# Seven instead of twelve attention steps ahead of the first matmul layer, and keys times values in four array quarters

## The reference, cut to what matters

```python
# q, k, v: 4 batches, 8 heads, 576 positions, 64 features; g_norm: 64
kv  = einsum('bhsd,bhse->bhde', k, v)            # 64 x 64 per head
out = einsum('bhsd,bhde->bhse', q, kv)
x   = out / sqrt(mean(out * out, -1) + 1e-6) * g_norm     # -> 2304 tokens x 512
x   = ((x @ w_a) * (x @ w_b)) @ w_out                      # layer 1, d_ff 1536
y   = (sigmoid(x @ w_gate) * (x @ w_val)) @ w_out2         # layer 2
```

## Time and profile before

| what | value |
|---|---|
| median of three runs | 886.71 us |
| profiled execution | 886.38 us, span of the trace 884.6 us |
| TensorE busy in the span | 870.4 us, 98% |
| VectorE busy | 646.0 us, 73% |
| ScalarE busy | 511.2 us, 58% |
| granted TensorE clock | full in all 40 slices |
| data moved | 189.81 MB, mean 215 GB/s |

### The profile page before, as it was taken

The page is one execution under the profiler, slowest core; times in us unless marked ns, Lnnn a source line. Parts: engine busy times, 40 slices in busy tenths (PEclk is TensorE's granted clock), DMA queues, the critical chain, the costliest instruction groups (busy, mean ns, idle before and its releaser), DMA issues.

```text
span 884.6 us, 16335 instructions
## 1 busy us (share of the span) xinstructions
PE 870.4 (98%) x5843; PEld 844.2 (95%) x5843; DVE 646.0 (73%) x1260; ACT 511.2 (58%) x1031; POOL 18.9 (2%) x69
## 2 busy tenths in 40 slices
PE   7999999999999999999999999999999999999998
PEld 5878999999999999999999999988999999999998
DVE  2688889872877893768994888982787894676773
ACT  3776655553565574555575556563666574656453
POOL 1122000000000000000000000000000000000000
PEclk9999999999999999999999999999999999999999
DMA  9843588886565682345583578788457486435276
GB/s 331 286 161 108 181 307 266 272 292 203 195 204 204 216 304 87 128 155 212 182 276 120 201 265 291 283 289 300 150 202 265 173 288 176 154 131 208 92 239 190
DMA packets 99344, 189.81 MB, mean 215 GB/s; under 512 B 6976, under 2 KB 48704, under 8 KB 99264
## 3 DMA queue, kind: packets, MB, share of 16 engines
q1 hardware_dynamic: 99184, 188.71, 63.4%
q10 hardware_dynamic: 80, 0.07, 0.0%
HBM read 146.28 MB, written 42.47 MB: 213 GB/s over the span
## 4 chain that ended last, share of the span: by engine, by line
PE 92%; DVE 3%; ACT 2%; DMA 1%; issue 1%; SPq 1%; POOL 0%; DVEq 0%; ACTq 0%; POOLq 0%
PE bank L893 58%; PE bank L979 10%; PE bank L977 10%; PE bank L929 6%; PE bank L932 4%; PE bank L828 1%; PE bank L805 1%; PE bank L791 1%; DMA q_in<-in_q_dram 1%; DMA wo<-wo_dram 1%; PE bank L841 1%; DVE x_lo L1429 1%; SPq L552 1%; ACT x_hi L1113 0%; DVE sum_sq L1325 0%
## 5 line engine op out<-in xcount | busy, mean ns | idle before, releaser
L893 PE MATMUL bank<-x_hi,w_hi 128*128 128x384 f32 x1008 | 340.1, 337 | 1.8 <-DVE c_a L1579 0.8
L893 PE MATMUL bank<-x_hi,w_lo 128*128 128x384 f32 x1008 | 337.9, 335 | 0.0
L893 PE MATMUL bank<-x_lo,w_hi 128*128 128x384 f32 x1008 | 337.4, 335 | 0.0
L893 PEld LDWEIGHTS bank<-x_hi,w_hi 128*128 128x128 f32 x1008 | 189.2, 188 | 7.3 <-issue 2.3
L893 PEld LDWEIGHTS bank<-x_lo,w_hi 128*128 128x128 f32 x1008 | 189.3, 188 | 2.3
L893 PEld LDWEIGHTS bank<-x_hi,w_lo 128*128 128x128 f32 x1008 | 189.2, 188 | 0.0
L1145 ACT ACTIVATE h_parts<-h 128x384 fp32r<-128x384 f32 x184 | 95.7, 523 | 81.3 <-PE bank L979 25.0
L1424 DVE TENSOR_TENSOR w_lo<-s_raw,w_hi 128x512 fp32r<-128x512 f32 x144 | 98.9, 687 | 50.2 <-ACT w_hi L1099 49.9
L1424 DVE TENSOR_TENSOR w_lo<-w_raw,w_hi 128x512 fp32r<-128x512 f32 (+1 forms) x144 | 79.5, 552 | 73.0 <-ACT w_hi L1099 73.0
L1465 DVE TENSOR_TENSOR h_parts<-h,h_parts 128x384 fp32r<-128x384 f32 x184 | 100.0, 552 | 22.3 <-ACT h_parts L1145 22.0
L1226 ACT ACTIVATE bank<-bank 128x384 f32<-128x384 f32 x72 | 34.2, 476 | 103.9 <-PE bank L893 103.9
(11 more groups left out here) (94 smaller groups left out, 822.6 us busy)
## 6 DMA issues: line engine op xcount, KB each, us to landing
wo<-wo_dram SPq DMA_DIRECT2D x60, 512.0 KB, 4.8
s_raw<-s_dram SPq DMA_DIRECT2D x48, 512.0 KB, 4.5
wo<-wo_sums_dram SPq DMA_DIRECT2D x48, 512.0 KB, 4.4
s_dram<-s_raw SPq DMA_DIRECT2D x24, 512.0 KB, 4.7
wo_dram<-wo SPq DMA_DIRECT2D x24, 512.0 KB, 5.3
wo_sums_dram<-h_parts SPq DMA_DIRECT2D x12, 1024.0 KB, 7.5
w_raw<-in_moe_w_a_dram SPq DMA_DIRECT2D x18, 512.0 KB, 3.6
w_raw<-in_moe_w_b_dram SPq DMA_DIRECT2D x18, 512.0 KB, 3.5
```

Source lines behind the costliest of these rows:

```text
L893: last = pe.matmul(to[:, 0:HT], w[:, u % 2, at, c, :], xx[:, i, c, :], start=(OPENS[i] and c == 0 and n_pass == 0), stop=(c == 1 and n_pas ...
```

## The change: what it does

1. Seven steps run in front instead of twelve. The thirteen others stand between the products of units 0 to 7, one every 15/4 slots. Keys times values of batches 2 and 3 move into slots 10 and 18 (`KV_LATE_AT`); their copies stand one slot later.
2. Keys times values takes two head pairs at a time and writes all four 64x64 quarters of the array: `tile_position=(i * DH, c * DH)` instead of `(i * DH, i * DH)`. There are as many matmuls as before. The copies are 64 wide in partition halves, four instructions per engine instead of two.
3. Loads: the weights of unit 0 come first of all, and are split first of all; batch 1's queries come in two parts; batch 3's keys and queries come in unit 0.
4. Unit 0 takes its products in the order 0, 3, 1, 2, 4, 5, 6; products 0 and 3 stand among the last back transposes of the seven steps. The operands are made in the same order.
5. The output steps of tile 0 start at unit 8 with two per unit, so ten first results are kept instead of four, the later ones in `t_raw`. The weight sums of tile 0 are three jobs instead of four, those of tile 1 three instead of two.

```diff
-    LATE = 12
-    KV_PIECE_AT = {0: ((0, 2),), 1: ((0, 3),), 2: ((1, 0),), 3: ((1, 1), (1, 2)), 4: ((1, 3),),
...
+    LATE = 7
+    KV_PIECE_AT = {1: ((0, 1),), 4: ((1, 0), (1, 1))}
...
+    QUERY_BEHIND = {1: (2, 3), 2: (4,), 4: (5, 6)}
+    X_BEHIND = {3: (0,), 4: (1,), 6: (2, 3)}
...
-    X_FIRST = (0, 3, 5, 1, 2, 4, 6)
-    T_SUMS_AT = {10: (0,), 11: (1,), LATE: (2,), LATE + 1: (3,)}
-    X_LO_AT = {8: (0,), 9: (3,), 10: (5,), 11: (1,), LATE: (2,), LATE + 1: (4,), LATE + 3: (6,)}
+    X_FIRST = (0, 3, 1, 2, 5, 4, 6)
+    T_SUMS_AT = {LATE + 1: (0,), LATE + 3: (1,), LATE + 4: (2,), LATE + 5: (3,)}
+    X_LO_AT = {5: (0,), LATE: (3,), LATE + 2: (1,), LATE + 3: (2,), LATE + 4: (4, 5), LATE + 5: (6,)}
...
-    QUERY_AT = {0: 12, 2: 13, 4: 14, 6: 15, 8: 16, 10: 17, 12: 18, 14: 19}
+    KV_LATE_AT = {10: 2, 18: 3}
+    QUERY_AT = {4 + 15 * n // 4: LATE + n for n in range(ALL_STEPS - LATE)}
+    ATTEND_AT = {k + 1: s for k, s in QUERY_AT.items()}
+    X_AT = {k + 5: s for k, s in QUERY_AT.items()}
+    OUT_FROM = 8
...
                 for r in range(R):
-                    for i in range(2):
-                        half = slice(i * DH, (i + 1) * DH)
-                        keys, values = [kv_in[half, pair_, which, r * DH:(r + 1) * DH] for which in range(2)]
-                        last = pe.matmul(kv_bank(b, i, pair_)[half, pair_ * DH:(pair_ + 1) * DH], keys, values,
-                                         start=(r == 0), stop=(r == R - 1), tile_position=(i * DH, i * DH))
+                    for c in range(2):
+                        for i in range(2):
+                            half = slice(i * DH, (i + 1) * DH)
+                            keys, values = [kv_in[half, 2 * group + c, which, r * DH:(r + 1) * DH] for which in range(2)]
+                            last = pe.matmul(kv_bank(b, i)[c * DH:(c + 1) * DH, group * DH:(group + 1) * DH], keys, values,
+                                             start=(r == 0), stop=(r == R - 1), tile_position=(i * DH, c * DH))
...
+            product(0, 0, 0)
+            transpose_x(LATE - 3)
+            transpose_x(LATE - 2)
+            product(0, 0, 3)
+            transpose_x(LATE - 1)
...
-        SUMS_AT = ({3: 0, 5: 1, 7: 2, 9: 3}, {1: 4, 4: 5}, {})
+        SUMS_AT = ({6: 0, 8: 1, 10: 2}, {1: 3, 3: 4, 5: 5}, {}, {3: 0, 5: 1, 7: 2, 9: 3}, {1: 4, 4: 5}, {})
```

More of the change, by code:

```diff
@@ L779, in transpose_q @@
                 b, group, quarter = place_of(s)
-                if not rest(s):
-                    pe.wait_ge(q_loaded[b % 2][group], 32 * (b // 2 + 1))
+                if b == 1:
+                    pe.wait_ge(q_loaded[1][0 if quarter == 0 and not rest(s) else 1], 16 * HEAD_PAIRS)
+                elif not rest(s):
+                    pe.wait_ge(q_loaded[b % 2][group], q_loads(b))
                 before = before_in_bank(qT_place, s)
@@ L1019, in _ @@
                         if i:
-                            for _ in range(2):
-                                next(behind, None)
-                    for _ in behind:
-                        pass
+                            for _ in range(2 * len(behind)):
+                                next(behind[(i - 1) // 3 * (len(behind) - 1)], None)
                 if fast(tau):
@@ L1070, in prepare @@
             def prepare(at):
-                for g in W_HI_AT.get(at, ()):
-                    split_w(0, g)
+                for u, g in W_HI_AT.get(at, ()):
+                    split_w(u, g)
                 for n in X_HI_AT.get(at, ()):
@@ L1193, in _ @@
             for s in range(LATE):
-                i = s % STEPS
+                if s:
+                    root(s - 1)
                 square(s)
-                if i + 2 < STEPS and s + 2 < LATE:
-                    copy_q(s + 2)
-                if i == STEPS - 1 and s + 1 < LATE:
-                    copy_q(s + 1)
-                root(s)
-                for b, pairs in KV_COPY_AT.get(s, ()):
-                    copy_kv(b, pairs)
-                if s >= LAG:
-                    write_x(s - LAG)
-                if i == STEPS - 1 and s + 2 < LATE:
-                    copy_q(s + 2)
-                prepare(s)
+                for ahead in X_BEHIND.get(s, ()):
+                    write_x(ahead)
+                prepare(s)
+                for b, groups in KV_COPY_AT.get(s, ()):
+                    copy_kv(b, groups)
+                for ahead in QUERY_BEHIND.get(s, ()):
+                    copy_q(ahead)
+            root(LATE - 1)
+            write_x(LATE - 3)
+            prepare(LATE)
+            seed(0, 0)
+            write_x(LATE - 2)
+            prepare(LATE + 1)
+            write_x(LATE - 1)
+            for i in range(2, FIRST):
+                prepare(LATE + i)
             for tau in range(ALL_TILES):
@@ L1528, in _ @@
                     invert(s - 1)
+                sum_squares(s)
                 prepare(s)
-                sum_squares(s)
-                for b, pairs in KV_COPY_AT.get(s, ()):
-                    copy_kv(b, pairs)
+                for b, groups in KV_COPY_AT.get(s, ()):
+                    copy_kv(b, groups)
                 if s:
                     normalise(s - 1)
+            invert(LATE - 1)
+            prepare(LATE)
+            prepare(LATE + 1)
+            normalise(LATE - 1)
+            for i in range(2, FIRST):
+                prepare(LATE + i)
             for tau in range(ALL_TILES):
```

395 lines of the change are left out of this document (239 added, 156 removed).

## The result

The changed kernel took 894.88 us (median of 4 runs, 893.7 to 898.77), the kernel before 886.56 us on the same chip (885.08 to 886.91): a ratio of 1.0105 (95% interval 1.0071 to 1.0138). The forecast was 887.0 us with a range of 882.5 to 892.5; the time is outside, on the slow side.

A forecast was written before the change was run, and what follows sets the result against it. TensorE was taken as bound, nearly without gaps, at full clock; some 10 of 886 us in play. 886.38 + 1.5 + 5.0 - 1.2 + 0.8 - 5.8 = 886.7 us, plus 0.33 for the median: 887.0 us, range 882.5 to 892.5.

The forecast's parts named there:

- four quarters, -5.8 us: Keys times values: four array quarters take 19 ns per record instead of 29.2, over eight 72-record pieces; between 0 and -8.4.
- the page cited in the prediction: Trainium skill page: some 60 cycles overhead per matmul, 25 ns, which would make the keys times values term -2.4 us.
- The relay: Unit 0's first products wait for operands handed on by VectorE and ScalarE, cover moved away; stage's gaps cost +5.0 us.
- Gaps 10.3 us: TensorE's summed waits from the first attend to product 6 of unit 0, against 5.3 us before.
- The prediction's second mechanism: VectorE and ScalarE set the pace of unit 0's first products once the steps covering them move; stage costs +5.0 us.
- The start, +1.5 us: Up to the first attend: unit 0's weights load ahead, so it starts at 12.8 us, before at 11.32.
- Units 8 on, at nothing: Later output steps in tile 0 were taken as hidden by units running from loaded weights, at no cost.
- +0.8 us between the products: Moved steps between products: slower matmuls behind transposes and waits for kv copies, less 0.5 us idle; +0.8 us.
- four quarters at full rate: Faster rival for keys times values: 14.6 ns per record, 884.4 us; chance 0.26.
- rate kept: Slower rival for keys times values: four quarters run no faster than two, 29.2 ns per record, 892.8 us; chance 0.15.

The follow-up runs named there:

- column halves apart: Changed kernel with keys times values run through its nine blocks for one pair, then the other, so never two column halves at work: 898.55 us, ratio 1.0123.
- third warm-up: Changed kernel with three wide warm-up matmuls in place of two ahead of the first piece of keys times values: 893.04 us, ratio 1.0073.
- changed again: The changed kernel run once more, unaltered: 896.35 us, ratio 1.0107; its profiled execution took 896.50 us.
- all three repairs: Changed kernel with third warm-up, 28 throw-away matmuls in the first products' gaps, and first two output steps split ahead of weight sums in unit 7: 892.71 us, ratio 1.0065.
- The filler: Changed kernel with 28 throw-away matmuls of 384 columns issued in the gaps of unit 0's first products: 894.54 us, ratio 1.0091.
- the run with a step inside the relay: Changed kernel with attention step 7 pulled into the gaps of unit 0's first products, later steps each one place earlier: 898.12 us, ratio 1.0128.

## Why the prediction was wrong

**The supply of instructions.** The step that failed most is "four quarters, -5.8 us". The rate was better than taken: 16.8 ns a record where 19 was chosen, which would have been (29.2 - 16.8) x 576 records = 7.1 us. What reaches the end is some 2 us in the changed kernel, by a difference that is not clear of noise (the run with column halves apart), and in the kernel before 1.6 us in the profiled execution and nothing in the median (888.23 against 886.64). Stops take back much of the rest, and they come from TensorE's own stream of instructions.

*Their place is a record number.* 2 records more moved them by 2, 28 by 28, 16 by 16. TensorE's records from its first one up to the stop, in the changed kernel, with the third warm-up and in the kernel before with four quarters (columns: busy us of TensorE, clock, DMA share, GB/s):

```profile
0.00:25.00 25.00, 17.20 (x343) 1.00 0.91 325
0.00:24.50 24.50, 18.45 (x343) 1.00 0.92 331
0.00:24.50 24.50, 18.42 (x343) 1.00 0.93 333
```

In eight of the profiles a stop stands behind exactly 343 records, in two different orders of the work, and the one in batch 2's piece behind 712, in all six profiles that have it. An instruction queue (q8) is in the trace, one packet of 16 KB at a time, and such a packet lies inside the long stop of the changed kernel's second profile (24.16 to 27.29 us; the window is 24.5 to 25.0 us):

```profile
q8 instruction: 1, 0.02, 12.0%
```

*Their end is the packet's.* Read from the traces, in us:

| kernel, stop behind | TensorE has run out | the packet starts | TensorE goes on | behind the packet's start |
|---|---|---|---|---|
| changed, 343 | 26.41 | 26.86 | 29.18 | 2.32 |
| changed again, 343 | 24.16 | 24.89 | 27.29 | 2.40 |
| third warm-up, 343 | 23.77 | 22.43 | 24.74 | 2.31 |
| all three repairs, 343 | 23.70 | 21.98 | 24.40 | 2.42 |
| all three repairs, 960 | 73.56 | 74.34 | 76.67 | 2.33 |
| kernel before, 843 | 51.58 | 50.19 | 52.48 | 2.29 |

The packets and the places come in step, one for one. Over the fourteen profiles the first eight packets belong to 27 stops called "issue", and each of these ends 2.1 to 2.8 us behind the start of its packet; where no stop stands, TensorE gets to the place 2.1 us or more behind it (the places of single records are good to a few). So the length of a stop is what is left of these 2.3 us or so when TensorE has run out. It is short where the packet started early (0.70 us) and long where it started only behind the last record (3.13 us). With column halves apart the packet starts at 22.85 us and TensorE reaches the place at 27.11: no stop. What decides when a packet starts, up to 0.8 us behind TensorE's last record, stays open.

From 343 to 712 records there are three packets, 123 records each. At 29.2 ns these last 3.6 us, at 16.8 ns 2.1 us (an estimate): two quarters leave the fetch enough time more often than four do. The kernel before has a single such stop, of 0.9 us, and the earlier trace rows show it as "L805 <- issue"; the prediction counted it among the waits and did not ask what it was. The Trainium skill (Runtime: NRT & Kernel Launch, Instruction fetch mechanics) calls the cost of crossing a 16 KiB block "mostly hidden", since an engine issues more slowly than it is refilled; the trace doesn't agree for these short matmuls, where the stops cost 0.5 to 3.1 us each. For the page cited in the prediction (the Trainium skill, TensorEngine Tiling (Array Packing), Instruction Overhead; 25 ns) the trace decides by what is counted: a record takes 16.8 ns, below it, and a matmul of the program, which is two records, 33.6 ns, above it.

**The clock.** The prediction took the full clock throughout and put no price on it. The rows of before gave no reason for another: there, attention steps fill the time. With them moved, gaps of up to 2.3 us stand between the products, and two or three products in each of the two profiles run at 1.2 GHz. In the run of 896.50 us these are product 2 (2.3 us in place of 1.3 to its end) and product 4 (2.1 in place of 1.15 to the next start); with the query transpose and product 5, which are slower in part, it makes 2.4 us; the 59 records behind the stop and the eight transposes after them add 1.4 us, of which some 0.7 would else have been spent waiting for `qT`. The filler took 1.8 us off the total, not all of it by the clock, and the third warm-up 3.3 us, of which the traces show only the shorter stop. The stops and the clock are not independent: in the second profile the clock falls behind the stop of 3.13 us.

**The relay, 0.9 us off.** "Gaps 10.3 us" was near: from the first attend to product 6 TensorE waited 12.2 us in the first profile, 9.4 without the stop of 2.77, with x_lo at the head of the list as worked out. The prediction's second mechanism stands; the run with a step inside the relay shows that VectorE and ScalarE set it.

**The start, +1.5 us.** The sum held in the one profile (12.8 us; 12.20 and 14.21 were measured), in part by luck: it counts the first piece at 2.25 us, which took 1.21 at full clock, while that piece starts at 8.4 and 8.7 us and not at 8.2, and the transposes and the warm-up take twice as long where TensorE is not at full clock.

**Units 8 on, at nothing.** Wrong by the 1.4 us wait at the first output step, out of 2.4 us of new idle time up to 240 us. The prediction had checked VectorE's load per unit, not the order inside one. Its "no waits over 0.3 us from unit 2 on" fails by this wait and by a stop of 1.38 us behind 959 records. The +0.8 us between the products were not measured by themselves.

**The account.** From 886.7 us for a profiled execution: 3.6 us of the quarters' gain not kept, 3.8 us of half clock, 2.4 us of idle time from 100 to 240 us, less 0.6 us at the start and 1.6 us of gaps (8.7 in that run, without the stop), make 894.3; the run has 896.5. The 2.2 us left are not assigned; they could be quarters' gain as well, since the 2.2 us taken as kept are 0.2 between the profiled executions. Of the rivals "four quarters at full rate" (14.6 ns) was about as near to the rate as the forecast, 16.8 ns lying between them, and "rate kept" nearest in time (892.8), for a reason that it did not name.

## What to carry to other kernels

When small matmuls get faster, ask what feeds them: here a stream of 16.8 ns records outran its own instructions, and a cheap way to find this out is to add a few records ahead and see whether a stop moves by as many. The DMA view then shows whether a packet of instructions started just before TensorE went on. Before moving work away from the gaps of a hand-over between engines, put a price on TensorE's clock as well: a gap costs its length and then up to the length of the work behind it. An engine's load per unit says little of one wait; the order of its list inside that unit does.

## What the runs showed of the hardware

- Four 64 x 64 quarters take 16.8 ns per record, two take 29.2, one takes 58 ns, in 160 records and in 16, under a clock column of 1.00. So one or two quarters take a record every 58 ns each, four one every 67 ns.
- TensorE went on behind a stop 2.1 to 2.8 us after a packet of 16 KB had started on the instruction queue, and a packet went with some 123 records.
- The profile's clock column can stay at 1.00 where everything takes twice as long: 0 to 11 us in the first profile, with transposes of 1.92 in place of 1.09 us up to 14.2 us. The trace's first entry on the clock is at 14.63 us there; ahead of it the column has nothing to go by.
- Throw-away matmuls in gaps of 1 to 2 us keep the granted clock at 1.00 where it was 0.56 on average.
- "Issue" stands for two things, an instruction that hasn't arrived and a load that is late (halts behind 85 and behind 72 records).
- Where the time of one kernel scatters, the longer executions can be those with the lower mean granted clock: in the kernel before with four quarters 886.54 to 890.11 us at 0.993 to 0.997, and 884.78 at 0.998.
